# Steps of a pair of heads reordered, casts and GpSimd's weight work moved, in an attention and two-layer kernel

## The reference

```python
scores = scale * np.matmul(q, k.transpose(0, 1, 3, 2))
bias = slopes[:, None, None] * (-np.abs(rel).astype(np.float32))[None, :, :]
mask = (rel >= 0) & (rel < window)                     # window = 128
scores = np.where(mask, scores + bias[None], -1000000000.0)
attn = np.exp(scores - np.max(scores, axis=-1, keepdims=True))
attn = attn / (np.sum(attn, axis=-1, keepdims=True) + 1e-09)
x = np.matmul(attn, v)                                 # then tokens x 512
g = (x @ w_in) * sigmoid(1.702 * (x @ w_in));  x = g @ w_out
g = (piecewise quadratic of x @ w2_in);        out = g @ w2_out
```

## Time and profile before

| | us |
|---|---|
| median of 3 runs | 909.62 (906.32 to 909.88) |
| the profiled execution | 911.26 |
| its span, first to last instruction | 909.4 |
| PE / DVE / ACT / POOL busy | 865.1 / 698.7 / 537.3 / 111.9 |
| PE waits for the attention's last pair until | 173.3 |
| the second duo of the feed-forward part begins | 209.4 |

### The profile page before, as it was taken

The page is one execution under the profiler, slowest core; times in us unless marked ns, Lnnn a source line. Parts: engine busy times, 40 slices in busy tenths (PEclk is TensorE's granted clock), DMA queues, the critical chain, the costliest instruction groups (busy, mean ns, idle before and its releaser), DMA issues.

```text
span 909.4 us, 15472 instructions
## 1 busy us (share of the span) xinstructions
PE 865.1 (95%) x5746; PEld 853.8 (94%) x5746; DVE 698.7 (77%) x980; ACT 537.3 (59%) x786; POOL 111.9 (12%) x83
## 2 busy tenths in 40 slices
PE   7898987689999999999999999999999999999998
PEld 6887887579999999999999999999999999999998
DVE  6567656256779887767799789797988879889794
ACT  3566665456767554667684355767555567766431
POOL 1578778200000000000000000000000000000000
PEclk8999998899999999999999999999999999999999
DMA  9876975025885746458776477178753761878821
GB/s 212 213 207 182 226 188 154 14 98 198 300 300 188 251 143 243 168 214 311 244 258 243 190 282 253 72 269 286 274 172 138 263 243 70 300 276 309 290 100 70
DMA packets 63064, 191.16 MB, mean 210 GB/s; under 512 B 7440, under 2 KB 14096, under 8 KB 59152
## 3 DMA queue, kind: packets, MB, share of 16 engines
q1 hardware_dynamic: 62992, 190.18, 62.1%
HBM read 117.81 MB, written 72.35 MB: 209 GB/s over the span
## 4 chain that ended last, share of the span: by engine, by line
PE 87%; issue 5%; ACT 4%; DVE 3%; DVEq 0%; ACTq 0%
PE ps L986 74%; PE ps L954 4%; PE ps L920 4%; PE ps L933 3%; ACT probs L1139 1%; PE ps L948 1%; PE ps L963 1%; ACT x_pairs L1154 1%; DVE wst L1509 1%; DVE w_first L1516 1%; PE ps L968 1%; ACT w_first L1184 1%; ACT probs_t L1159 0%; DVE arena L1563 0%; DVE probs L1477 0%
## 5 line engine op out<-in xcount | busy, mean ns | idle before, releaser
L986 PE MATMUL ps<-arena,w_first 128*128 128x384 f32 x1764 | 332.1, 337 | 3.7 <-ACT ps L1246 2.5
L986 PEld LDWEIGHTS ps<-arena,w_first 128*128 128x128 f32 x1764 | 310.6, 188 | 5.9 <-issue 4.6
L986 PE MATMUL ps<-arena,w_rest 128*128 128x384 f32 x1260 | 241.0, 337 | 1.1 <-ACT ps L1226 0.8
L986 PEld LDWEIGHTS ps<-arena,w_rest 128*128 128x128 f32 x1260 | 220.1, 188 | 2.3 <-issue 1.7
L1563 DVE TENSOR_TENSOR arena<-raw_first,arena 128x768 fp32r<-128x768 f32 (+1 forms) x116 | 150.7, 1312 | 77.6 <-ACT arena L1197 77.5
L1197 ACT ACTIVATE arena<-raw_first 128x768 fp32r<-128x768 f32 (+1 forms) x120 | 131.9, 1117 | 48.6 <-DVE raw_first L1548 39.5
L986 PE MATMUL ps<-w_rest,arena 128*128 128x256 f32 x945 | 132.5, 281 | 0.0
L986 PEld LDWEIGHTS ps<-w_rest,arena 128*128 128x128 f32 x945 | 121.1, 189 | 0.1
L1477 DVE CUSTOM_DVE_ANT_0 probs<-ps,bias_sb 128x256 f32<-128x256 f32 (+1 forms) x128 | 44.8, 387 | 56.9 <-PE ps L920 50.8
L986 PE MATMUL ps<-w_first,arena 128*128 128x256 f32 x567 | 88.0, 282 | 0.0
L1563 DVE TENSOR_TENSOR arena<-raw_rest,arena 128x1536 fp32r<-128x1536 f32 (+1 forms) x48 | 71.3, 1486 | 12.0 <-ACT arena L1197 11.9
(11 more groups left out here) (110 smaller groups left out, 980.3 us busy)
## 6 DMA issues: line engine op xcount, KB each, us to landing
gd<-g SPq DMA_DIRECT2D x24, 1536.0 KB, 6.0
raw_rest<-gd SPq DMA_DIRECT2D x32, 768.0 KB, 5.2
qk_raw<-qkT SPq DMA_DIRECT2D x62, 288.0 KB, 4.9
wst<-w_pairs SPq DMA_DIRECT2D x32, 512.0 KB, 6.1
raw_first<-gd SPq DMA_DIRECT2D x16, 768.0 KB, 6.0
yd<-ust SPq DMA_DIRECT2D x6, 1536.0 KB, 6.3
wd<-ust SPq DMA_DIRECT2D x4, 1536.0 KB, 8.6
raw_first<-yd SPq DMA_DIRECT2D x4, 1536.0 KB, 6.9
```

What stands on the lines that cost most here:

```text
L986: last = nc.tensor.matmul(to, stationary, moving, start=start and n == 0, stop=n == len(steps) - 1, skip_group_check=True)
```

## The change

- **Order of steps.** `ITEMS` is regrouped and a pair now runs its steps in the order 2, 3, 0, 1, 4. The first step uses the even head alone, the fourth is the even head's last, the last uses the odd head alone. PE waits for the even head's split before the pair's first step and for the odd head's before its second. The even head's cast moves from DVE's iteration 5q+4 to 5q+3, the odd head's from 5q+7 to 5q+6 (with the slot's previous pair q).
- **Lags.** Two of a pair's four value steps and the transposes of the tails come one step later.
- **POOL.** It splits all heads from 2 on and the second pieces of heads 0 and 1. Weight work is put behind earlier heads, `sum_s1` behind head 24 instead of 26, its last operand behind head 29, and S3 and S4 are added behind head 31.
- **ACT.** `round_both(0)` and `(1)` go from steps 27 and 45 to 17 and 32, set 2 from the first duo to step 48, the operands from 60, 66, 74, 76 to 54, 57, 66, 67, and S3, S4 to 76 and 78. SP's load of weight set 2 goes from q = 10 to q = 8.
- **First two heads.** Both are loaded in two pieces; DVE casts and splits the first pieces, ACT casts the second and POOL splits them. The first pair's order is 2, 4, 3, 0, 1. The bias table comes in two loads.

```diff
-ITEMS = ((), ((0, 0), (1, 0)), ((0, 1), (0, 2)), ((0, 3), (1, 1)), ((1, 2), (1, 3)))
-FIRST_ORDER = (2, 3, 4, 0, 1)
-ORDER = [(q, d) for q in range(PAIR_COUNT) for d in (FIRST_ORDER if q == 0 else range(STEPS))]
+ITEMS = ((), ((0, 0), (1, 0)), ((0, 1), (0, 2)), ((0, 3), (1, 3)), ((1, 1), (1, 2)))
+
+
+STEP_ORDER = (2, 3, 0, 1, 4)
+FIRST_ORDER = (2, 4, 3, 0, 1)
+ORDER = [(q, d) for q in range(PAIR_COUNT) for d in (FIRST_ORDER if q == 0 else STEP_ORDER)]
...
-DVE_HEADS = (0, 1, 3)
...
-VALUE_LAG = 4
+VALUE_LAG = (None, 4, 5, 5, 4)
+DRAIN = 4
 WRITE_LAG = 5
 PAIR_LAG = 6
 COPY_LAG = 7
-PAIR_TAIL_LAG = 8
-COPY_TAIL_LAG = 9
+PAIR_TAIL_LAG = 9
+COPY_TAIL_LAG = 10
 X_STORE_LAG = 6
-ODD_LAG = 3
...
-EARLY = 4
+
+EARLY = 6
...
+    def last_use(head):
+
+        return max(m for m, (q, d) in enumerate(ORDER) if q == head // 2 and
+                   (d == 0 or any(e == head % 2 for e, _ in ITEMS[d])))
...
+        def load_piece(e, first):
+            if e == 0:
...
             for half in range(2):
-                sp.dma_start(both_first(qk_raw[half * DIM:(half + 1) * DIM, 0])[:, :, cols],
-                             qkT[0].rearrange("p (t s) -> p t s", t=2)[:, :, cols]).then_inc(first_in if first else qk_in[0], 16)
+                sp.dma_start(piece(qk_raw, e, first)[half * DIM:(half + 1) * DIM],
+                             source_piece).then_inc(first_in[e] if first else qk_in[e], 16)
...
-        load_first_operands(True)
-        sp.dma_start(distance[:], bias_table).then_inc(distance_in, 16)
-        load_first_operands(False)
+        load_piece(0, True)
+        sp.dma_start(distance[:, 0:BAND], bias_table[:, 0:BAND]).then_inc(distance_in, 16)
+        load_piece(1, True)
+        load_piece(0, False)
+        load_piece(1, False)
         sp.dma_start(ident[:], identity).then_inc(ident_in, 16)
-        for h in range(1, HEADS):
+        sp.dma_start(distance[:, BAND:], bias_table[:, BAND:]).then_inc(tail_distance_in, 16)
+        for h in range(2, HEADS):
             load_operands(h)
-            load_values(h - 1)
+            load_values(h - 2)
+        load_values(HEADS - 2)
         load_values(HEADS - 1)
...
-            if q == 10:
+            if q == 8:
                 load_weights(2)
             if q == 13:
                 load_first_x(1)
...
+        def split_rest(e):
+
+            pool.wait_ge(rest_rounded, e + 1)
+            nc.gpsimd.tensor_tensor(piece_lo(e, False), piece_keys(qk_raw, e, False), f32(piece_keys(qk_hi, e, False)),
+                                    ALU.subtract).then_inc(qk_split[e], 1)
+            pool.wait_ge(qk_split[e], 1)
+            if e == 0:
+                nc.gpsimd.tensor_tensor(piece_queries(qk_hi, e, False), piece_queries(qk_raw, e, False),
+                                        f32(piece_queries(qk_hi, e, False)), ALU.subtract).then_inc(qk_split[e], 1)
+                pool.wait_ge(qk_split[e], 2)
+
         def split_head(head):
...
+        def sum_s3():
+            nc.gpsimd.tensor_tensor(quadrant(0, 1, 0), quadrant(0, 0, 0), quadrant(0, 1, 0), ALU.subtract).then_inc(sums_made, 1)
+            pool.wait_ge(sums_made, 3)
+
+        def sum_s4():
+            data_in(pool, 0, 0, 1)
+            nc.gpsimd.tensor_tensor(combined(0), quadrant(0, 0, 1), combined(0), ALU.subtract).then_inc(sums_made, 1)
+            pool.wait_ge(sums_made, 4)
...
+        split_rest(0)
+        split_rest(1)
         for head in range(2, 2 * PAIR_COUNT):
-            if head not in DVE_HEADS:
-                split_head(head)
-            if head in (9, 10, 11):
-                add_weights(0, head - 9)
+            split_head(head)
+            if head in (7, 8, 9):
+                add_weights(0, head - 7)
+            if head in (10, 11, 12):
+                split_weights(0, head - 10)
             if head in (13, 14, 15):
-                split_weights(0, head - 13)
+                add_weights(1, head - 13)
             if head in (16, 17, 18):
-                add_weights(1, head - 16)
-            if head in (20, 21, 22):
-                split_weights(1, head - 20)
-            if head in (23, 24, 25):
-                add_weights(2, head - 23)
+                split_weights(1, head - 16)
+            if head in (19, 20, 21):
+                add_weights(2, head - 19)
+            if head == 24:
+                sum_s1()
+            if head == 25:
+                split_operand(A11)
             if head == 26:
-                sum_s1()
+                split_operand(S1)
             if head == 27:
-                split_operand(A11)
+                sum_s2()
             if head == 28:
-                split_operand(S1)
+                split_operand(S2)
             if head == 29:
-                sum_s2()
-            if head == 30:
-                split_operand(S2)
-        split_operand(A12)
+                split_operand(A12)
+        sum_s3()
+        sum_s4()
+        split_operand(S3)
+        split_operand(S4)
...
         def scores(m):
             q, d = ORDER[m]
-            if (q, d) == (0, 2):
-                pe.wait_ge(first_split, 2)
-            elif q == 0:
-                for head in (0, 1):
-                    pe.wait_ge(qk_split[head], 2)
-            elif d == 0:
-                for head in (2 * q, 2 * q + 1):
-                    pe.wait_ge(qk_split[head % SPLIT_RING], 2 * (head // SPLIT_RING) + 2)
+            if q == 0:
+                if d in (2, 4):
+                    pe.wait_ge(first_split[0 if d == 2 else 1], 2)
+                elif d == 3:
+                    for head in (0, 1):
+                        pe.wait_ge(qk_split[head], splits(head))
+            elif d in (2, 3):
+                head = 2 * q if d == 2 else 2 * q + 1
+                pe.wait_ge(qk_split[head % SPLIT_RING], splits(head))
...
-                if last_step == m - VALUE_LAG:
+                if last_step == m - VALUE_LAG[ORDER[last_step][1]]:
                     weigh_values(gi)
...
         def make_bias(pair):
 
-            act.wait_ge(distance_in, 16)
             for h in (2 * pair, 2 * pair + 1):
                 nc.scalar.activation(bias_sb[:, h], distance[:, 0:BAND], ACT.Copy, scale=SLOPES[h]).then_inc(bias_made, 1)
+                if pair == 0:
+                    round_rest(h)
+            if pair == 0:
+                act.wait_ge(tail_distance_in, 16)
             nc.scalar.activation(bias_tail[:, pair], distance[:, BAND:BAND + TAIL_KEYS], ACT.Copy,
                                  scale=SLOPES[2 * pair]).then_inc(bias_made, 1)
+
+        def round_rest(e):
+
+            act.wait_ge(qk_in[e], 32)
+            nc.scalar.activation(piece(qk_hi, e, False), piece(qk_raw, e, False), ACT.Copy).then_inc(rest_rounded, 1)
...
         act.wait_ge(cleared, CLEARED)
+        act.wait_ge(distance_in, 16)
         make_bias(0)
...
-            if m in (1, 6, 11):
-                make_bias((1, 6, 11).index(m) + 1)
+            if m in (3, 6, 11):
+                make_bias((3, 6, 11).index(m) + 1)
             if (q := pair_at(m, COPY_LAG)) is not None:
                 copy_pair(q)
-            if m == 27:
-                round_both(0)
-            if m == 45:
-                round_both(1)
-            if m in (60, 66, 74, 76):
-                round_operand(0, (A11, S1, S2, A12)[(60, 66, 74, 76).index(m)])
+            if m in (17, 32, 48):
+                round_both((17, 32, 48).index(m))
+            if m in (54, 57, 66, 67, 76, 78):
+                round_operand(0, (54, 57, 66, 67, 76, 78).index(m))
...
-            if c == 0:
+            if c == 0 and u:
                 round_weights(w + 2, 0)
             copy_d(D, 0)
-            round_operand(k, S3)
-            if c == 0:
+            if k:
+                round_operand(k, S3)
+            if c == 0 and u:
                 round_weights(w + 2, 1)
             seed_c(D)
             copy_d(D, 1)
-            round_operand(k, S4)
+            if k:
+                round_operand(k, S4)
             round_operand(k, A22)
...
+        def round_first(e):
+
+            dve.wait_ge(first_in[e], 32)
+            nc.vector.tensor_copy(piece(qk_hi, e, True), piece(qk_raw, e, True)).then_inc(first_rounded, 1)
+            dve.wait_ge(first_rounded, e + 1)
+            nc.vector.tensor_tensor(piece_lo(e, True), piece_keys(qk_raw, e, True), f32(piece_keys(qk_hi, e, True)),
+                                    ALU.subtract).then_inc(first_split[e], 1)
+            nc.vector.tensor_tensor(piece_queries(qk_hi, e, True), piece_queries(qk_raw, e, True),
+                                    f32(piece_queries(qk_hi, e, True)), ALU.subtract).then_inc(first_split[e], 1)
...
             nc.vector.tensor_copy(loaded(qk_hi, head), loaded(qk_raw, head)).then_inc(qk_rounded, 1)
-            if head in DVE_HEADS:
...
-        round_first(True)
-        round_first(False)
-        for m in range(ALL_STEPS + COPY_TAIL_LAG):
+        round_first(0)
+        for m in range(ALL_STEPS + COPY_TAIL_LAG - 1):
```

(43 more changed lines are left out.)

67 lines of the change are left out of this document (34 added, 33 removed).

## The result

The changed kernel takes 898.8 us (median, 896.7 to 900.4), the kernel before on the same chip 909.55 us: ratio 0.9888, 95% interval 0.9856 to 0.9921. The gain is 10.8 us; forecast were 18.4. The time lies outside the forecast of 886.5 to 896 and at the upper end of the wide range, 881 to 899. The profiled execution took 899.89 us, its span is 898.0. In the table, X stands for the start of POOL's first sum of x.

A forecast was written before the change was run, and what follows sets the result against it. PE binds from the second duo on, unchanged; ahead of it PE waits for POOL's splits and sums. Gains of 15.6 us to step 79 and 2.8 in the first duo, 18.4, give 891.2 us by the median; forecast 886.5 to 896, range 881 to 899.

The forecast's parts named there:

- Start: First two heads' smaller pieces and moved splits: 3 us gained, step 10 at 28.5 instead of 31.55.
- Chain 1: ACT's rounding of weight set 0 at step 17 waits for POOL's sums; PE loses 1.1 us in step 20.
- Chains 2 and 3: ACT's roundings at steps 32 and 48 wait for POOL's sums; PE loses 4.5 us in step 35, 2.8 in step 50.
- x: POOL stands 8.3 us in sum_s1 behind head 24 for x, landing at 125.7; PE loses 5.1 us in step 60.
- From X on: From x's landing to step 76, POOL's operations, heads and five casts at 0.7 us bind: 35.8 us, step 76 at 161.5.
- First duo: PE's waits of 2.49 and 0.27 us behind ACT's copy and for S4's remainder go: 2.8 us gained.
- The sum: 15.6 us up to step 79 plus 2.8 in the first duo: 18.4 off, profiled execution at 892.9 us.
- x in time: Rival: SP gets x there 8 us sooner, no new wait, another 7.6 us gained: 883.6 us; chance 0.20.
- Casts that cost nothing: Rival: DVE's casts take no POOL time, instead of 0.7 us each; some 8 us more, 883 us; chance 0.06.
- PE alone: Rival: all waits go and PE binds at 1.74 us a step, step 75 at 141.6: 873 us; chance 0.05.
- Waits that stay, moved: Rival: PE waits at the second step and within steps for ACT, POOL's backlog recurs in every chain: 900 us; chance 0.12.
- The clock: Rival: PE's clock stays low behind waits in steps 21 to 50; kernel slower, needing 22.9 us lost; chance 0.04.

The follow-up runs named there:

- after: The changed kernel with all parts of the change, against the kernel before: 898.8 us, ratio 0.9888.
- run 12: Changed kernel with POOL's and ACT's weight and operand work put back, S2 rounded at step 71, and weight set 2's load back at q = 10: 880.7 us.
- run 10: Kernel before with the new order of steps alone and S2 rounded at step 71 instead of 74: 883.7 us, ratio 0.970.
- Run 1: Changed kernel with weight set 0 loaded before the operands of heads 8 and 9 instead of behind them: 891.5 us, ratio 0.980.
- Run 3: Changed kernel with the even head's cast one DVE iteration later, behind the division of the finished pair: 898.8 us, ratio 0.987.
- run 4: Changed kernel with set 0 loaded earlier, x stored and loaded a pair earlier, and the even cast behind the division: 884.7 us, ratio 0.972.
- run 5: Kernel of run 4 with the casts of even heads from 4 on made by ACT instead of DVE: 884.7 us, ratio 0.972.
- run 6: Changed kernel with S3, S4 and weight set 2's rounding and splitting back in the first duo: 901.9 us, ratio 0.991.
- run 11: Changed kernel with POOL's and ACT's work on the three weight sets alone put back, operands left as changed: 894.0 us, ratio 0.980.
- run 9: Changed kernel with POOL's and ACT's weight and operand work put back, but S2 rounded at step 71 and set 2, S3, S4 ahead of the first duo: 886.5 us.
- before: The kernel without the change, 909.55 us on the same chip beside the changed kernel.

## Why the prediction was off

**What bounds the kernel.** Right: the second duo to the end is the same, and everything happens ahead of it.

**Start.** Taken as 3 us, measured 5.8 at step 10. It is worth nothing in the end: in after POOL stands 6.99 us for set 0 soon behind it. Where that wait is absent the lead is lost too: runs 12 and 10 (with and without the new start) have step 10 at 25.66 and 27.35 but step 20 at 45.38 and 45.27.

**Chain 1, the step that failed.** The prediction has for set 0 "head 9 cast at 41.3, split 44.3, added 45.1" and looked only at heads and casts. Of each moved piece of POOL's work it asked when POOL would come to it, but for weight set 0 not when its data would be there, though it asked just this for x. The set landed at 31.49 + 10.4 = 41.9, the last addition ended at 51.21, PE lost 5.56 us instead of 1.1, and step 21 came 6.2 us later than forecast. Run 1 settles it: with the transfer earlier, step 21 comes 5.1 us earlier and the kernel gains 8.0 us more.

**Chains 2 and 3.** Forecast 4.5 and 2.8 us. In after no wait of this kind over 1 us stands there (0.82 in step 35, none in step 50). In their place a pair takes 9.27 us (step 30 at 72.40, step 35 at 81.67) instead of 8.7, with waits as those of 1.51 and 0.96 us above: the even cast stands ahead of the division that PE waits for. This edit had been costed at nothing, with nothing said of what is queued behind the cast. Steps 36 to 60 took 44.7 us where 44.5 were forecast: that is luck, two errors that cancel. Run 3 shows one of the chains under it: without the division's waits, PE waits 3.65 us for exponentials in step 35, where 4.5 were forecast; in step 50 it still waits under 1 us, where 2.8 were.

**x.** The wait was right in kind, place and size (9.05 and 5.02 us for 8.3 and 5.1); POOL's first sum of x began 1.4 us later behind step 60 than forecast.

**From X on.** 35.8 us forecast, 35.75 measured (134.07 to 169.82), yet by a sum in which one term is wrong. The casts were priced at 0.7 us each. The row behind it showed POOL idle for 0.76 us, but it waited then for that cast's own data. The second support, 9.0 us over heads 13 to 23, was of the same kind: 8.2 of them are eight such waits of 0.76 to 1.55 us. Where POOL has other work ready a cast costs it 0.4 us, by runs 4 and 5. After has five such operations in the stretch, 2.2 us in all instead of 3.5, and step 76 began 1.35 us behind head 31's split. Here too the total is right by errors that cancel. The Trainium skill, page "SBUF — State Buffer", section "Who interferes with whom", says that GpSimd and a two-port DVE operation lock each other out for a whole instruction. Runs 4 and 5 agree with the exclusion, and give its price here; the cast, 0.75 us alone, was done 0.61 to 0.65 us behind POOL's operation, so that it shuts POOL out for its whole length is not shown.

**First duo.** 2.8 us forecast; from step 79 to the second duo it is 22.8 us instead of 26.9, 4.1 less, and run 6 puts this part at 3.4 us by that stretch and at 1.7 us by the medians.

**The sum.** Up to X 8.4 us later than forecast, the first duo 1.3 us better: 892.9 + 7 is the 899.89 us of the profiled execution.

**The rivals.** x in time (883.6, 7.6 us for the wait) was about the right price for a real reserve: run 4, which has it beside the edits of runs 1 and 3, takes 884.7 us, 6.8 less than run 1. Casts that cost nothing: 0.4 us each. PE alone: not reached by any run, the best is 880.7. Waits that stay, moved (900) gave nearly the time, but by luck: a transfer did it, not a backlog of POOL. The clock: it was 0.61 from 50 to 56 us, with the wait of step 20, 0.73 from 56 to 60 and full from 60 on, which made the two steps from 55.04 to 60.00 some 1.4 us longer than two calm ones (4.96 instead of 3.5). The mechanism is there, and far from the 22.9 us that the rival needed. Its condition, "a wait of 2.4 us and more", does not hold: the slow steps that it quotes stood behind a wait of 1.75 us, and in after the clock was 0.50 from 86 to 88 us behind two waits of 0.91 and 0.82 us, which made step 36 1.2 us longer.

**What the prediction did not ask.** Whether the parts help or hinder each other. The new order alone gains 21.4 us, and the parts beside it take half of that away. Undone one after the other, they give back 6.9 us (the work on the weights, run 11), 7.5 more (the operands' work, run 9) and 6.1 more (set 2's transfer, run 12), 20.5 in all. Another order of undoing might divide the sum otherwise: in after itself no cast behind set 2's issue (76.21) waits over 1 us for its load, as two do in run 9. Run 10 has this work where before had it, but for S2's rounding, and needs it no earlier: PE waits there for no weight sum. A sum made once for the order alone and once for all would have shown which part carries the gain.

**Left over.** Run 12's step 76 is 2.9 us later than run 10's (151.89 and 149.00), though both round S2 at step 71. The profiles show a difference of the clock between. PE waited 2.27 us at 137.72 in run 12 and 2.21 us at 137.38 in run 10, for divided heads; PE busy, granted clock, DMA share, GB/s from 138 to 146 us, of run 12 and then of run 10:

```profile
138.00:142.00 4.00, 4.00 (x21) 0.50 0.21 80
142.00:146.00 4.00, 4.00 (x28) 0.68 0.00 0
```

```profile
138.00:142.00 4.00, 4.00 (x39) 1.00 0.21 78
142.00:146.00 4.00, 4.00 (x38) 1.00 0.00 0
```

Run 12 ran at 1.2 GHz behind the wait, run 10 at 2.4. S2's rounding began at 146.05 instead of 142.69, and POOL, which has no such wait in run 10, stood for it:

```profile
147.04 1.83 POOL L926 TENSOR_TENSOR arena<-raw_first,arena 128x768 fp32r<-128x768 f32 x1 [3.05 <-ACT arena L1274]
```

That the clock is the cause is argued from these rows, not shown by an edit. Whether it falls there in every execution of run 12 stays open; only one of each was profiled, and run 6 shows that profiles of equal work can differ by as much.

## What to carry over

When work is moved ahead on an engine that works in order, ask of every piece when its data land, not only when the engine comes to it: a piece that comes too early stops all that is queued behind it. Undo a compound change part by part, since the part that works may be worth more alone; here the order alone gave 21.4 us, and the whole change 10.8. Give a wait the price of what is bound behind it: 8.2 us less idle time on POOL brought 7 us or more, though PE stood only 5.

## What the runs showed of the hardware

- A DVE cast of 128x1152 (0.75 us alone) that was issued beside a POOL operation ended 0.61 to 0.65 us behind that operation, and the POOL operation shown from that moment took 0.4 us longer (1.41 to 1.81, 1.83 to 2.22). Seven of seven in run 4, four of four in run 5.
- In after, weight set 0 (512 KB) landed 10.4 us after its issue at 31.49 and set 1, of the same size, 5.0 us after its issue at 54.5.
- In run 9, behind one issue of 512 KB at 74.50, two casts stood 2.44 and 1.91 us for the loads of their heads; with that issue two pairs later (run 12) neither wait is there, and the kernel gained 6.1 us more.
- Two waits of PE of nearly the same length in nearly the same place (2.27 and 2.21 us) were followed by a granted clock of 0.50 in one kernel (run 12) and of 1.00 in the other (run 10), and two waits under 1 us (0.91 and 0.82) by 0.50 in after.
